# First expert's weights on one DMA queue: eight 256 KB pieces of w1 during attention, w2 in one transfer behind the last q and k

## The reference, cut to what matters

```python
logits = np.einsum('bsd,de->bse', x, w_gate)
local_gate = 1.0 / (1.0 + np.exp(-np.einsum('bsd,de->bse', x, w_local).squeeze(-1)))
...
            fresh_e = int(np.argmax(logits[b, s]))
            if s == 0 or local_gate[b, s] < 0.5:
                e = fresh_e
            else:
                e = prev_e if prev_e >= 0 else fresh_e
...
            h = np.maximum(x[b, s] @ w1[e], 0.0)
            out[b, s] = p[e] * (h @ w2[e])
```

## Time and profile before

| | us |
|---|---|
| median of three runs | 497.78 (497.13 to 498.15) |
| profiled execution, its own time | 500.14 |
| its span, first to last instruction | 498.3 |
| PE busy in the span | 463.3 (93%) |
| DVE, ACT, POOL busy | 263.2, 221.7, 193.4 |
| mean clock granted to PE, as a share of full | 0.951 |

### The profile page before, as it was taken

The page is one execution under the profiler, slowest core; times in us unless marked ns, Lnnn a source line. Parts: engine busy times, 40 slices in busy tenths (PEclk is TensorE's granted clock), DMA queues, the critical chain, the costliest instruction groups (busy, mean ns, idle before and its releaser), DMA issues.

```text
span 498.3 us, 13006 instructions
## 1 busy us (share of the span) xinstructions
PE 463.3 (93%) x4148; PEld 374.6 (75%) x4155; DVE 263.2 (53%) x419; ACT 221.7 (44%) x393; POOL 193.4 (39%) x248
## 2 busy tenths in 40 slices
PE   7999899899989468999999999999999999999981
PEld 4888788688868335788888888888888888888860
DVE  5788868548866686254353452435346464522220
ACT  3787677547766103245254252525527282422210
POOL 7877757547886002122204213331321515132200
PEclk9999989759999767999999999999999999999996
DMA  8999999965116576306416511551646555120100
GB/s 177 194 199 203 224 216 209 198 149 113 28 43 151 142 240 188 33 33 228 148 67 232 172 62 54 199 169 64 218 160 235 161 233 168 75 74 32 34 26 6
DMA packets 86033, 69.23 MB, mean 139 GB/s; under 512 B 47982, under 2 KB 71022, under 8 KB 86000
## 3 DMA queue, kind: packets, MB, share of 16 engines
q1 hardware_dynamic: 81504, 57.78, 43.2%
q0 software_dynamic: 4496, 11.03, 7.2%
HBM read 59.34 MB, written 10.76 MB: 141 GB/s over the span
## 4 chain that ended last, share of the span: by engine, by line
PE 82%; SPq 6%; DVE 5%; issue 3%; ACT 1%; DMA 1%; POOL 0%; DVEq 0%; POOLq 0%; ACTq 0%
PE psum L1456 52%; PE psum L1474 4%; PE psum L1192 4%; PE psum L1174 3%; PE psum L1265 2%; PE psum L1280 2%; PE psum L1434 2%; PE psum L1358 2%; PE psum L1228 2%; SPq L329 2%; SPq L356 2%; PE psum L1202 2%; PE psum L1368 1%; PE psum L1294 1%; PE psum L1251 1%
## 5 line engine op out<-in xcount | busy, mean ns | idle before, releaser
L1456 PE MATMUL psum<-w_ring,xg_t 128*128 x552 | 133.9, 398 | 2.3 <-DVE xg_t L1113 1.6
L1456 PE MATMUL psum<-w_ring,h_t 128*128 x552 | 134.3, 398 | 1.7 <-issue 1.7
L1456 PEld LDWEIGHTS psum<-w_ring,xg_t 128*128 128x128 f32 x552 | 102.3, 189 | 24.9 <-issue 2.7
L1456 PEld LDWEIGHTS psum<-w_ring,h_t 128*128 128x128 f32 x552 | 101.9, 188 | 24.8 <-issue 2.0
L631 POOL DMA_INDIRECT out<-tile_bufs,to_row x23 | 23.5, 1024 | 193.8 <-DVE tile_bufs L1128 193.8
L1101 DVE TENSOR_TENSOR w_ring<-w_ring (+1 forms) x28 | 63.0, 2290 | 26.2 <-ACT w_ring L781 26.2
L781 ACT CAST w_ring<-w_ring (+1 forms) x28 | 52.1, 1908 | 32.9 <-DMA w_ring<-moe_w 32.9
L802 ACT ACTIVATE tile_bufs<-psum 128x512 f32<-128x512 f32 x46 | 25.0, 595 | 87.6 <-PE psum L1456 87.6
L1113 DVE TENSOR_TENSOR xg_t<-psum,xg_t 128x512 fp32r<-128x512 f32 x24 | 16.6, 690 | 83.7 <-ACT xg_t L795 83.7
L809 ACT CAST h_t<-psum 128x512 fp32r<-128x512 f32 x46 | 24.8, 591 | 74.1 <-PE psum L1474 74.1
L1128 DVE TENSOR_SCALAR tile_bufs<-psum,slot_w 128x512 f32<-128x512 f32 x23 | 17.2, 749 | 56.9 <-PE psum L1456 51.9
(11 more groups left out here) (181 smaller groups left out, 638.5 us busy)
## 6 DMA issues: line engine op xcount, KB each, us to landing
w_ring<-moe_w SPq DMA_DIRECT2D x14, 2048.0 KB, 8.7
early<-q SPq DMA_DIRECT2D x32, 144.0 KB, 3.6
early<-k SPq DMA_DIRECT2D x32, 144.0 KB, 3.7
early<-v SPq DMA_DIRECT2D x16, 288.0 KB
x_rows<-early SPq DMA_DIRECT2D x48, 96.0 KB, 2.5
w_ring<-moe_w SPq DMA_DIRECT2D x8, 512.0 KB, 6.8
early<-v SPq DMA_DIRECT2D x32, 120.0 KB
early<-v SPq DMA_DIRECT2D x64, 13.5 KB
```

Of the source, the lines that this page charges most:

```text
L1456: ins = mm(bank[b][:, :], rows, w_ring[:, bass.ds(at + (off + c * width + n * 512), 512)], start=(c == 0 and k == 0), stop=(c == chunks - ...
```

## The change

The pieces of the first expert's w1 become half as large (half the columns of a 128-row chunk, 256 KB): one follows `two_units(kk)` for kk = 2 to 5, two for kk = 6 and 7, and the loop over kk is written out to its end. w2 is one transfer of 2 MB behind the loads of the last units, ahead of the gate weights. The semaphore now counts nine transfers. The split by ACT and POOL keeps its steps, its order and its place.

```diff
-            def load_first(i):
-                at = WCOLS + i * FCOL
-                if at < WCOLS + W1C:
-                    n = FCOL // F
-                    src, c, shape = w1v, i * n, dict(c=n)
-                else:
-                    n = FCOL // D
-                    src, c, shape = w2v, (at - WCOLS - W1C) // D, dict(c=n)
-                sp.dma_start(w_ring[:, at:at + FCOL].bitcast(F32).rearrange("p (c n) -> p c n", **shape),
-                             src[0, :, c:c + n, :]).then_inc(s_first_in, 16)
+            def load_first_w1(c, half):
+                n = F // 2
+                at = WCOLS + c * F + half * n
+                sp.dma_start(w_ring[:, at:at + n].bitcast(F32), w1v[0, :, c, half * n:(half + 1) * n]
+                             ).then_inc(s_first_in, 16)
+
+            def load_first_w2():
+                sp.dma_start(w_ring[:, WCOLS + W1C:2 * WCOLS].bitcast(F32).rearrange("p (c d) -> p c d", c=KF),
+                             w2v[0, :, :, :]).then_inc(s_first_in, 16)
...
-            for kk in range(2, 2 + FPIECES // 2):
-                two_units(kk)
-                load_first(2 * kk - 4)
-                load_first(2 * kk - 3)
-            with sp.Fori(2 + FPIECES // 2, UNITS // 2) as kk:
-                two_units(kk)
+            for kk in range(2, UNITS // 2):
+                two_units(kk)
+                if kk < 2 + KD:
+                    load_first_w1(kk - 2, 0)
+                else:
+                    load_first_w1(2 * kk - 4 - 2 * KD, 1)
+                    load_first_w1(2 * kk - 3 - 2 * KD, 1)
+            load_first_w2()
...
-                act.wait_ge(s_first_in, 16 * FPIECES)
+                act.wait_ge(s_first_in, 16 * (2 * KD + 1))
```

## The result

| | before | changed |
|---|---|---|
| median of 20 runs, us | 497.96 (493.58 to 506.61) | 492.93 (489.20 to 495.57) |
| profiled execution, its own time | 500.14 | 491.42 |
| its span | 498.3 | 489.6 |
| mean clock granted to PE | 0.951 | 0.968 |

The change makes the kernel faster: the ratio is 0.9919, 95% interval 0.9891 to 0.9947. (The ratio leaves out executions over 1.5% above their kernel's fastest, which only the kernel before has here, so the medians lie further apart than the ratio says.) The forecast was 486.3 us. The time lies inside the range given, 484.3 to 493.0, but only by 0.07 us, and outside the 484.5 to 488.5 of the forecast's own case; the gain is 5 us by medians (4 by the ratio) and not 11.7.

The account below looks back on a forecast made before the run. PE was bound by late q loads beside w1 pieces and the low clock after; 500.14 - 12.74 + 0.5 = 487.9 for the profiled execution, 485.5 or 487.9 as median, forecast 486.3 us, range 484.3 to 493.0.

Parts of the forecast that it names:

- the forecast's own case: PE no longer waits for q, w2 costs little: 486.3 us, 484.5 to 488.5, chance 64%.
- room of q: Time from the end of SP's issue of a unit's q to PE's need; 7.6 at unit 4, 6.0 at unit 12.
- The 404 GB/s row: Weights' rate with a full queue; priced 0.79 MB less per round at 1.95 us, rather than 3.3 at 241 GB/s.
- the 7.6 us that I had as a ceiling: Room at unit 4; more was held impossible at unit 12, as the buffers come free no earlier.
- the +0.5 us for w2: Cost of 2 MB of w2 behind the last q and k, ahead of unit 14's windows; bounds 0 to 4 us late.
- the landing of the windows of unit 14 at 116.9: These v windows, queued behind w2 (landing 115.2), land 0.4 us before PE's local values of unit 14 need them at 117.3.
- the second rival: w2 holds up unit 14's windows by 1 to 4 us, PE idles, its clock falls: 488 to 496, say 491; 13%.
- The term of -12.74 us: Whole excess of the bodies of units 7, 11 and 12: 3.6 us waiting for q, 9.1 of low clock.
- the two cases: Profiled execution's extra 2.4 us over the median lies elsewhere (485.5) or in these same stalls (487.9).
- A price by count: Rival: each w1 piece costs 2 us whatever its size, so one stall returns: 488.3 to 494.6, say 491; 17%.
- The 2.0 us and the 2.6 us: For the count rival: fixed cost of a DMA beside bytes / 436 GB/s, and the resulting cost of a 256 KB piece.
- The slower outcome: Third rival: unit 14's windows land after 123.7, making the kernel slower, about 500 us; 6%.

Follow-up runs that it names:

- the second profile: The changed kernel, unaltered, timed and profiled again as reference for the first group of experiments: median 493.05 us, ratio 0.9926, span 492.1.
- w2 last: Against the changed kernel, w2 issued behind the v windows of units 14 and 15, on its own semaphore awaited only by its split steps: median 489.06 us, ratio 0.9853.

## Why the prediction was right or wrong

**Right: the cause and the cure of the waits for q.** The room of q falls by the bytes of weights beside it. With 0.26 MB a round no q was late, and the bodies ran at 7.14 us, as forecast. The loss of room was 0.4 us a round by the sum and none in the trace (8.1 us at unit 4, 8.2 at unit 12, 6.0 expected); the second profile lost 0.15 a round (7.4 to 6.8). The 404 GB/s row was a cautious price, and the 7.6 us that I had as a ceiling wasn't one.

**Wrong, first: the +0.5 us for w2.** The step that failed is the landing of the windows of unit 14 at 116.9. PE could start only at 119.77, in the second profile at 121.44, and the last body grew by 3.0 us in the one and 5.9 in the other; in the medians, the changed kernel against w2 last, it is 4.0 us. This is the second rival, at 13%. I had let SP issue the windows in 3.1 us behind w2, from a place where the queue wasn't backed up, and had started the queue empty at 100.6, though its engines had been full for long. The trace shows SP held for 12.1 us and w2 landing at 105.45 + 11.3 = 116.8, 1.6 after the expected 115.2. The rule I had named beside it, that descriptors of one queue start in ring order on each engine (the Trainium skill, DMA: Bandwidth & Descriptors, queues, rings and completion order), is not what costs: the run with w2 on ACT's queue shows that another queue doesn't help. A second section of that page, that issuing engines are not separate DMA queues, says so: all run on the same 16 engines and interleave. The trace agrees (3.1 us of wait with w2 on ACT's queue).

**Wrong, second: the size of what was removed.** The term of -12.74 us was right for the profiled execution: 11.87 of it came back, and 0.80 was given away by a later start, since the body of unit 7 began at 60.33 and not 59.53. But as a gain of medians it was too large. With every wait gone (w2 last) the median is 9.7 us below that of before in the same group, 489.06 against 498.80, and by the ratio of 0.9853 it is 7.3 us. I had seen that the profiled execution lay 2.4 us above the median and forecast a time between the two cases; the runs give the difference to these stalls. They also show why: how the waiting is split, and how long the clock stays low behind it, change from one execution to the next.

Together: the forecast of 486.3 stands for 12.0 us of stalls (497.78 + 0.5 - 486.3). 3.5 us too little for w2 and 2.3 too much for the stalls make 5.8 of the 6.6 us between 486.3 and 492.93. The other 0.8 us is no more than the median of before moved between groups (497.78 to 498.80). That the time fell inside the range is owed to the width taken in for the rivals, not to the sum.

**The rivals.** A price by count is refuted (sixteen pieces, no wait). The 2.0 us and the 2.6 us worked out from them are, in the Trainium skill (DMA: Bandwidth & Descriptors, the anatomy of one DMA), a fit for transfers issued by GpSimd, and these are issued by SP; no run here shows such a price. The slower outcome didn't come: PE's wait for the windows ended at 119.8 and 121.4, not after 123.7.

**What each part of the change gives**, by medians: moving w2 out of the rounds seems most of it, 498.19 to 491.04, when w2 goes where nobody waits. Lighter rounds of w1 add 1.3 to 2.5 us (489.70 and 488.52); by means, in which the five longer executions of the run with only w2 moved count, it is about half and half: 497.9, 493.5, then 489.5 and 488.5. The piece size adds nothing in itself. Where the change put w2 it gives 4 us back.

Four of the versions tried clearly beat both kernels: w2 last with w1 in eight pieces of 256 KB (489.06), four of 512 KB (488.52) or sixteen of 128 KB (489.70), and half of w2 last (489.37). The order among them is not settled, since the first and the fourth were timed on other occasions than the other two.

## What to carry to other kernels

A prefetch that isn't urgent belongs behind the last transfer that is, not just behind the last one of the kind that used to be late; list everything that is still due, with its due time, and add the bytes of the prefetch at the rate of a full queue to each. The wait on it should be as narrow as its use: a semaphore of its own for w2 was what made the late place possible. And when a profile shows short waits followed by a low clock, take the gain of removing them from several executions, for one profile's share of low clock is a draw. Look at the length of each wait before the sum: in these runs three waits of 3.7 us in all cost 5.6 us, and two of 3.6 us in all cost 12.7.

## What the runs showed of the hardware that I had not expected

The same wait of 1.36 us at the same point cost 3.19 us in one execution and 8.70 in another, through the time that PE's clock stayed at 1.2 GHz though PE was busy (9.94 of 9.94 us in the second body, at a mean granted clock of 0.66). With w2 last and the light rounds, the six executions of each version agree within 1.2 to 3.2 us (256, 512 and 128 KB pieces: 1.2, 1.7, 3.2); twelve and twenty of the changed kernel spread over more than 6, and the 17 to 29 of the kernel before over 12.5 to 15.4. More executions spread further by themselves, so a part of the difference may come from their number alone.

SP's issue of a transfer, some 0.35 us each where nothing is in the way, is held for up to 3 us while the DMA engines work through a large transfer. A large transfer that another engine issued holds it too, but less: the windows of units 14 and 15 take 12.7 us to be issued with w2 on ACT's queue (108.27 to 120.95) and 8.3 with w2 last. What holds it (a limit on what is outstanding, in which unit) was not tried.
